# Three-stage kernel (decayed attention, two gated layers): the 256-token tile as last of each layer

## The reference

```python
# q, k, v: (4, 8, 576, 64); gamma = 1 - 2**(-5 - head)
Dmat = np.where(rel >= 0, gamma ** rel, 0.0)        # rel = i - j
attn = (q @ k.T / sqrt(64) * Dmat) @ v
x = attn.transpose(0, 2, 1, 3).reshape(2304, 512)
h = x @ w_in                                        # (512, 2048)
g = np.where(h >= 1, h, np.where(h <= -1, 0.0, (h + 1) ** 2 / 4))
x = g @ w_out                                       # (2048, 512)
out = ((x @ w_a) * (x @ w_b)) @ w_out2              # (512, 1536), (1536, 512)
```

## Time and profile before

| | |
|---|---|
| median of 3 runs | 920.28 us (919.37 to 922.73) |
| profiled execution, its own time | 922.37 us |
| span, first to last instruction | 920.3 us |
| mean granted PE clock | 0.997 |
| PE busy | 905.1 us (98%) |
| DVE busy | 349.1 us (38%) |
| ACT busy | 285.0 us (31%) |
| POOL busy | 36.4 us (4%) |

### The profile page before, as it was taken

One profiled execution on the slowest core, in us unless ns is written; L12 is line 12 of the kernel. 1 busy time (PEld: TensorE's weight loads), 2 busy tenths in 40 slices (PEclk: granted clock), 3 DMA queues, 4 the chain that ended last, 5 costly groups with the idle time before them and its releaser, 6 DMA issues.

```text
span 920.3 us, 12089 instructions
## 1 busy us (share of the span) xinstructions
PE 905.1 (98%) x5160; PEld 767.9 (83%) x5160; DVE 349.1 (38%) x565; ACT 285.0 (31%) x476; POOL 36.4 (4%) x54
## 2 busy tenths in 40 slices
PE   7989999999999999999999999999999999999998
PEld 6978888888899888888888888888899888888886
DVE  4666665434445433555653212211221311131112
ACT  1235545333445433445542212111211211121111
POOL 4541000000000000000000000000000000000000
PEclk9999999999999999999999999999999999999999
DMA  7989000000000000022320000100010000010001
GB/s 277 317 297 349 0 1 1 1 1 0 1 2 1 1 1 1 0 69 86 121 103 1 1 1 1 47 0 1 1 46 2 23 1 1 1 45 1 1 1 46
DMA packets 20053, 42.46 MB, mean 46 GB/s; under 512 B 1568, under 2 KB 12320, under 8 KB 20000
## 3 DMA queue, kind: packets, MB, share of 16 engines
q1 hardware_dynamic: 19424, 40.90, 12.9%
q10 hardware_dynamic: 576, 0.79, 0.3%
HBM read 36.97 MB, written 4.72 MB: 45 GB/s over the span
## 4 chain that ended last, share of the span: by engine, by line
PE 95%; DMA 2%; POOL 1%; issue 1%; DVE 0%; SPq 0%; ACT 0%; POOLq 0%
PE score_a L382 5%; PE score_b L382 5%; PE score_b L384 5%; PE score_a L384 5%; PE score_b L383 5%; PE score_a L383 5%; PE score_a L330 4%; PE kv_b L347 4%; PE score_a L331 4%; PE kv_b L348 4%; PE score_b L331 4%; PE ret_b L348 4%; PE score_b L330 4%; PE ret_b L347 4%; PE score_a L332 4%; PE ret_b L349 4%
## 5 line engine op out<-in xcount | busy, mean ns | idle before, releaser
L499 DVE TENSOR_TENSOR gate_w<-relu_s,relu_r 128x512 f32<-128x512 f32 (+1 forms) x80 | 51.1, 638 | 131.9 <-ACT relu_r L612 131.9
L384 PE MATMUL score_a<-xh,w_all 128*128 128x512 f32 (+1 forms) x240 | 88.3, 368 | 0.0
L384 PE MATMUL score_b<-xh,w_all 128*128 128x512 f32 (+1 forms) x240 | 88.3, 368 | 0.0
L383 PE MATMUL score_a<-xl,w_all 128*128 128x512 f32 (+1 forms) x240 | 88.3, 368 | 0.0
L383 PE MATMUL score_b<-xl,w_all 128*128 128x512 f32 (+1 forms) x240 | 88.3, 368 | 0.0
L382 PE MATMUL score_a<-xh,w_all 128*128 128x512 f32 (+1 forms) x240 | 88.2, 368 | 0.0
L382 PE MATMUL score_b<-xh,w_all 128*128 128x512 f32 (+1 forms) x240 | 88.2, 368 | 0.0
L621 ACT ACTIVATE gh<-gated 128x512 fp32r<-128x512 f32 (+1 forms) x80 | 47.2, 590 | 104.9 <-DVE gated L502 104.9
L528 DVE TENSOR_TENSOR gated<-score_a,relu_s 128x512 f32<-128x512 f32 (+1 forms) x30 | 19.1, 638 | 156.9 <-ACT relu_s L641 156.9
L508 DVE TENSOR_TENSOR gl<-gated,gh 128x512 fp32r<-128x512 f32 (+1 forms) x80 | 51.1, 638 | 50.8 <-ACT gh L621 50.6
L528 DVE TENSOR_TENSOR gated<-score_b,relu_s 128x512 f32<-128x512 f32 (+1 forms) x30 | 19.1, 637 | 126.6 <-ACT relu_s L641 126.6
(11 more groups left out here) (107 smaller groups left out, 1934.9 us busy)
## 6 DMA issues: line engine op xcount, KB each, us to landing
kq<-k_q SPq DMA_DIRECT2D x16, 576.0 KB, 6.1
w_raw<-w SPq DMA_DIRECT2D x12, 768.0 KB, 4.1
kvt<-kv_tok SPq DMA_DIRECT2D x16, 512.0 KB, 4.8
w1a_raw<-w SPq DMA_DIRECT2D x12, 512.0 KB, 6.3
out<-x_all SPq DMA_DIRECT2D x18, 256.0 KB, 3.0
w1b_raw<-w SPq DMA_DIRECT2D x4, 512.0 KB, 6.6
decays<-decays_c ACTq DMA_DIRECT2D x4, 193.5 KB, 7.0
vtail<-v_tail SPq DMA_DIRECT2D x16, 32.0 KB, 4.8
```

The lines of the kernel that those rows point to most:

```text
L383: pe.matmul(o, w2_slab(f, 0)[:, at], xl[:, k, 0:WIDTHS[t]], start=False, stop=False)
L384: mm = pe.matmul(o, w2_slab(f, 1)[:, at], xh[:, k, 0:WIDTHS[t]], start=False, stop=(k == KT - 1))
L499: nc.vector.tensor_tensor(gate_w[:, 0:WIDTHS[t]], relu_s[:, 0:WIDTHS[t]], relu_r[:, 0:WIDTHS[t]], ALU.add).then_inc(gatew_ready, 1)
```

## The change

The 256 tile moves from third to last place of the one table, so in both layers:

```diff
-WIDTHS = (TC, TC, TC // 2, TC, TC)
+WIDTHS = (TC, TC, TC, TC, TC // 2)
```

## The result

The changed kernel takes **927.35 us** (median of 7 runs, 925.58 to 929.43) against 920.28 (7 runs). The ratio is **1.0077, 95% interval 1.0062 to 1.0092**: 0.8% slower. The profiled execution took 928.65 us with a span of 926.7.

What follows compares the result with a forecast made beforehand. PE, busy 98% of the span, was taken as the bound, with time set by matmul columns, which the change keeps. Terms +7.35 - 2.35 + 0.9 = +5.9 us gave a median of 926.2 us, range 922.5 to 929.5.

Steps and rivals of the forecast that it cites:

- Boundaries at 0: Passing between tiles of 512 and 256 columns in new places was to cost PE nothing: 0 us.
- The walk, +7.35: Layer 1's last tile, step by step: slab steps of 4.44 us against PE's 2.88 make PE wait, 7.35 us lost.
- the links: Delays between dependent ACT and DVE instructions, read from the trace: 4.44 us per slab step, 2.12 per plain step.
- Rival A: Layer 1's last tile: slab work hidden, as busy shares suggest; only the tail's gain remains, 917.9 us; 6%.
- rival B: Layer 1's last tile: slab work partly hidden, slab step 3.5 to 4.1 us, result within 0.5%; 17%.
- DMA not in it: Slab loads in layer 1's last tile land in time, so DMA adds no wait.
- The clock, +0.9: End of layer 1: PE's idle makes its clock fall once, costing 0 to 1.7 us, middle 0.9.
- Rival C: PE's clock swings through layer 1's stalled stretch, adding 5.1 and 1.7 us, to 932; 7%.
- The tail, -2.35: End of layer 2: shorter last chain saves 0.98 us and fewer last copies 1.37, together 2.35 us.

Runs made afterwards that it cites:

- e4_interleaved: Changed kernel with the same slabs at the same steps, rounded and subtracted inside the gate instead of behind it; 920.51 us, ratio 0.9999 to the kernel before.
- e2_layer2_last: Kernel before with the 256 tile last in layer 2 only, layer 1 keeping it third; 920.22 us, ratio 0.9997.
- e3_spread: Changed kernel with four slabs fewer in layer 1's narrow last tile, moved to layer 2's first tile; 920.47 us, ratio 0.9998 to the kernel before.
- e6_fourth: Kernel before with the 256 tile moved to fourth place in both layers, last tiles 512 wide; 920.83 us, ratio 1.0008.
- a2_changed_again: The changed kernel itself, measured once more beside the filled kernels; 928.32 us, ratio 1.0081 to the kernel before.
- e1_layer1_last: Kernel before with the 256 tile last in layer 1 only, layer 2 keeping it third; 928.44 us, ratio 1.0084.
- e5_one_less: Changed kernel with one slab less in the pace-setting stretch of layer 1's last tile; 925.73 us, ratio 1.0066 to the kernel before.
- e7_filled: Changed kernel plus 14 unread matmuls where PE idles at the end of layer 1; 926.92 us, ratio 1.0076 to the kernel before.
- e8_filled_one_less: Changed kernel with one slab less in the pace-setting stretch, plus the same 14 unread matmuls; 925.48 us, ratio 1.0057 to the kernel before.

## Why the prediction held, and the term that didn't

Forecast 926.2 (922.5 to 929.5), measured 927.35. The mechanism of the loss is the one forecast; the gain set against it was not there. The range is wide enough to hold the sum with that gain or without it, so the time alone would not have told. Step by step:

- *Boundaries at 0*: right. The fourth-place kernel repeats both stages to 0.03 us, and the hole at the start of the 256 tile is there in it too (0.2 us at 343.81).
- *The walk, +7.35*: 7.14 us. Six slab steps were 0.02 and two plain ones 0.03 shorter than the links say, which is 0.18 of the 0.21. Rival A (hidden, by busy shares) and rival B (a step of 4.0) fall with the rows above. A needed a slab step of 3.2 us or less: e4_interleaved has 2.88, the order of the changed kernel 4.42.
- *DMA not in it*: right. No DMA stands among PE's or ACT's waits in that stretch, and the slabs landed in 4.3 us at the median.
- *The clock, +0.9*: 0.68 in the profiled execution, and 2.8 where a double fall lay almost wholly on matmuls, above the 1.7 of my bounds. I had not seen why the single fall is cheap: 1.9 of its 3.4 us lie on project(14), behind which PE would have waited 0.9 us for the relu anyway. Rival C (a swinging clock) did not come: each trace has one fall at that place, of 3.4 or 6.8 us. The shorter waits of 0.5 to 1.3 us ahead of it left the clock at 1.00. The trace before had said as much, which the prediction overlooked: behind its one fall the attention pauses again, for 1.07 us up to 64.91, at clock 1.00. The Trainium skill (TensorE: Matmul & The Clock Gate, "A second HAM failure mode") tells of a clock that goes up and down with frequent short idles between matmul groups. These traces don't show that: they have one fall, behind the longest pause.
- *The tail, -2.35*: **wrong, it is about 0**. I took the chain from relu_s and the copies to be shorter, which they are (by 0.96 and 1.36 us), and forgot two things: that the output matmuls stay the same in number, and that the copies of the earlier blocks run while PE makes the later ones. Before, 24 output matmuls stand behind the last products, 12 of them while the chain runs; after, 12, of which 6 while it runs. The 12 others (2.72 us) have moved ahead of the last products. The 3.6 us from the last copy to the end, taken to be the same in both, became 3.1. The right sum counts idle time only: PE now waits 0.61 + 0.11 us more than its pace ahead of the last outputs and lost 0.24 + 0.10 before, and the time behind the last matmul goes from 4.72 to 4.22 us: +0.38 - 0.50 = -0.1 (the 0.7 in the expectation was read less exactly). e2_layer2_last measures the term alone at -0.3 us, interval -1.4 to +0.7.

With the walk at 7.14, the tail at -0.1 and the clock at 0.7 the sum is +7.7 us, against +7.85 in the traces from the first hidden matmul on. The forecast of +5.9 is 1.2 us under the medians' +7.1: the tail made it 2.3 too low, walk and clock 0.4 too high, and the medians lie 0.8 under the two traces, within their scatter.

No experiment beats the kernel before: e2_layer2_last, e3_spread, e4_interleaved and e6_fourth equal it within their intervals. PE has no idle there that the order of the tiles could win.

## What to carry to other kernels

When a fixed-size piece of work rides on the steps of a loop, ask what the step costs on the chain through all engines that share it, and compare that with the bound engine's step at the narrowest tile it can meet; that the added busy time still fitted (24.9 of 28.6 us) said nothing here. If the chain is too long, there are two remedies, which came out equal here: move the work to a wider tile, or keep it where it is and interleave it. The side work belongs where its engine would wait, not behind the link that others wait for. And where one engine is bound from end to end, count only its idle time; work that leaves the tail turns up ahead of it.

## What the runs showed of the hardware

- One pause of PE (2.7 us by the modelled end of the matmul before it, 3.0 from start to start) was followed by a fall of its clock to half, for 3.4 us in two traces (after, a2_changed_again) and 6.8 us in two others (e1_layer1_last, e5_one_less), with nearly the same program. Waits of 0.5 to 1.3 us shortly ahead of it left the clock at 1.00. With 14 filler matmuls in the pauses it stayed up in both traces that had them (e7_filled, e8_filled_one_less).
- What such a fall costs depends on where it lies: 0.68 us of 3.4 where a wait for another engine follows within it, 2.8 us of 6.8 where nearly all of it lies on matmuls that wait for nothing.
- Two engines that take turns on one chain can hold PE up although neither is full: a step took 4.42 us with the slab behind the gate and 2.88 with the same work inside it.
